# Waiting for a low part at the third matmul of a chunk in a three-layer kernel

## What is computed

```python
def _moe_ref(x, w_gate, w1, w2):
    ...                          # greedy assignment of 384 tokens to each expert
    for e in range(E):
        mask = assigned == e
        h = np.maximum(x[mask] @ w1[e], 0.0)
        out[mask] = h @ w2[e]

def _moe2_ref(x, w_gate, w_val, w_out):
    g = x @ w_gate
    silu = g * (1.0 / (1.0 + np.exp(-g)))
    val = x @ w_val
    return (silu * val @ w_out).astype(np.float32)
```

## Time and profile before

| | |
|---|---|
| median of 3 runs | 854.0 us (853.72 to 854.21) |
| the profiled execution | 853.57 us, span 851.7 us |
| TensorE busy | 821.5 us, 96% of the span, 6116 matmuls |
| TensorE weight loads busy | 784.0 us, 92% |
| VectorE, ScalarE, GpSimd busy | 508.2 us (60%), 299.1 us (35%), 235.7 us (28%) |
| of the 85.50 us from 273.00 to 358.50 (one expert's turn) | TensorE 85.35, weight loads 83.67, VectorE 48.11, ScalarE 28.05, GpSimd 22.03; granted clock 1.00 |
| largest shares of the chain that ended last | `ps_up` L1775 48%, `ps_acc` L1775 28% |

### The profile page before, as it was taken

One profiled execution on the slowest core, in us unless ns is written; L12 is line 12 of the kernel. 1 busy time (PEld: TensorE's weight loads), 2 busy tenths in 40 slices (PEclk: granted clock), 3 DMA queues, 4 the chain that ended last, 5 costly groups with the idle time before them and its releaser, 6 DMA issues.

```text
span 851.7 us, 16768 instructions
## 1 busy us (share of the span) xinstructions
PE 821.5 (96%) x6116; PEld 784.0 (92%) x6116; DVE 508.2 (60%) x1095; ACT 299.1 (35%) x607; POOL 235.7 (28%) x263
## 2 busy tenths in 40 slices
PE   9999993899999999999999999999999999999995
PEld 5888882699999999999999999999999999999995
DVE  9999987746554655465546554655466546642332
ACT  2566652432343234322432333233323332333221
POOL 3222210388613041304130413041305040504001
PEclk9999996899999999999999999999999999999998
DMA  8898852402300230023002300230023002300000
GB/s 292 280 328 286 288 174 77 147 1 75 103 27 1 74 102 20 8 74 102 18 9 74 102 18 9 74 102 18 9 74 102 18 9 74 102 19 11 0 1 32
DMA packets 25858, 70.98 MB, mean 83 GB/s; under 512 B 3808, under 2 KB 10464, under 8 KB 25824
## 3 DMA queue, kind: packets, MB, share of 16 engines
q1 hardware_dynamic: 19296, 56.39, 20.2%
q0 software_dynamic: 3072, 9.44, 3.4%
q10 hardware_dynamic: 3456, 4.72, 1.5%
HBM read 61.10 MB, written 9.44 MB: 83 GB/s over the span
## 4 chain that ended last, share of the span: by engine, by line
PE 80%; DVE 2%; ACT 1%; issue 1%; POOLq 0%; POOL 0%; DVEq 0%; ACTq 0%
PE ps_up L1775 48%; PE ps_acc L1775 28%; PE ps_up L1868 1%; PE ps_turn_again L1002 1%; PE ps_turn_again L1023 1%; PE ps_turn L1781 1%; DVE z_low L1720 1%; ACT z_high L1654 0%; PE ps_turn_again L840 0%; DVE quick_at_row L922 0%; DVE quick_at_row L809 0%; PE ps_up L1781 0%; POOLq L1908 0%; DVE x_low L1761 0%; DVE quick_base L822 0%
## 5 line engine op out<-in xcount | busy, mean ns | idle before, releaser
L1775 PE MATMUL ps_up<-z_high,gated_high 128*128 128x384 f32 x576 | 197.8, 343 | 1.5 <-DVE z_low L1720 1.5
L1775 PE MATMUL ps_up<-z_high,gated_low 128*128 128x384 f32 x576 | 195.0, 339 | 0.0
L1775 PE MATMUL ps_up<-z_low,gated_high 128*128 128x384 f32 x576 | 192.9, 335 | 0.0
L1560 POOL TENSOR_TENSOR w_low<-w_raw,w_high 128x384 fp32r<-128x384 f32 x120 | 118.5, 1013 | 251.3 <-ACT w_high L1641 251.0
L1775 PEld LDWEIGHTS ps_up<-z_high,gated_high 128*128 128x128 f32 x576 | 108.2, 188 | 3.0 <-issue 2.1
L1725 DVE TENSOR_TENSOR act_out<-ps_up,act_out 128x384 f32<-128x384 f32 x96 | 53.4, 556 | 92.4 <-ACT act_out L1657 90.7
L1775 PEld LDWEIGHTS ps_up<-z_high,gated_low 128*128 128x128 f32 x576 | 108.3, 188 | 0.0
L1775 PEld LDWEIGHTS ps_up<-z_low,gated_high 128*128 128x128 f32 x576 | 108.1, 188 | 0.0
L1660 ACT CAST u_high<-ps_up 128x384 fp32r<-128x384 f32 x96 | 46.0, 479 | 169.6 <-DVE ps_up L1729 169.6
L1657 ACT ACTIVATE act_out<-ps_up 128x384 f32<-128x384 f32 x96 | 47.1, 490 | 144.8 <-PE ps_up L1775 144.8
L1775 PE MATMUL ps_acc<-gated_high,u_high 128*128 128x384 f32 x288 | 97.3, 338 | 0.3 <-DVE u_low L1732 0.3
(11 more groups left out here) (220 smaller groups left out, 1420.3 us busy)
## 6 DMA issues: line engine op xcount, KB each, us to landing
w_raw<-in_experts SPq DMA_DIRECT2D x64, 384.0 KB, 3.0
qka_in<-in_qka SPq DMA_DIRECT2D x22, 770.5 KB, 5.7
gated_raw<-in_gated SPq DMA_DIRECT2D x12, 576.0 KB, 6.2
v_in<-in_v SPq DMA_DIRECT2D x24, 192.0 KB, 5.2
x_rows<-y_rows ACTq DMA_DIRECT2D x24, 192.0 KB, 4.4
qka_in<-in_qka SPq DMA_DIRECT2D x2, 512.0 KB, 4.7
qka_in<-in_qka SPq DMA_DIRECT2D x2, 258.5 KB, 3.4
out<-o_tok,to_rows POOLq DMA_INDIRECT x24
```

Source lines behind the costliest of these rows:

```text
L1560: part = pool.tensor_tensor(w.low[:, m % RING, cols], w.raw[:, m % RING, cols], w.high[:, m % RING, cols].bitcast(F32), ALU.subtract)
L1775: mm = pe.matmul(acc, lhs[a], rhs[b], start=(first and i == 0), stop=(last and i == 2))
```

## The change

Before, each place that reads a split operand for the first time waits for both of its parts ahead of the first of the three matmuls. After, it waits for the high part there, and `product` waits for the low part ahead of the third matmul, which is the only one to read it. This holds for x at the three slices of up(0), for h at each down chunk, for z at the three slices of the first gate chunk, and for u at each projection chunk. In the projection u stands on the left, where its low part was read by the second matmul; there the second and the third matmul change places (`low_of == "lhs"`). The values and what is summed stay as they are.

```diff
@@ -1769,9 +1769,12 @@
             expert(E - 1, last=True)
 
         def tensor(pe):
-            def product(acc, lhs, rhs, first, last):
-
-                for i, (a, b) in enumerate(((0, 0), (1, 0), (0, 1))):
+            def product(acc, lhs, rhs, first, last, low_of, low_ready=None, count=None):
+
+                parts = ((0, 0), (1, 0), (0, 1)) if low_of == "rhs" else ((0, 0), (0, 1), (1, 0))
+                for i, (a, b) in enumerate(parts):
+                    if i == 2 and low_ready is not None:
+                        pe.wait_ge(low_ready, count)
                     mm = pe.matmul(acc, lhs[a], rhs[b], start=(first and i == 0), stop=(last and i == 2))
                 return mm
 
@@ -1785,19 +1788,19 @@
                 for k in range(K1):
                     if m == 0:
                         pe.wait_ge(x_high_ready, K1 * e + k + 1)
-                        pe.wait_ge(x_low_ready, K1 * e + k + 1)
                     cols = slice(k * P, (k + 1) * P)
                     mm = product(ps_up[m % 2][0][:, 0:CAP], (w.high[:, m % RING, cols], w.low[:, m % RING, cols]),
-                                 (x_high[:, k, :], x_low[:, k, :]), k == 0, k == K1 - 1)
+                                 (x_high[:, k, :], x_low[:, k, :]), k == 0, k == K1 - 1, "rhs",
+                                 x_low_ready if m == 0 else None, K1 * e + k + 1)
                 mm.then_inc(h_ready, 1)
 
             def down(e, m):
                 pe.wait_ge(h_high_ready, FC * e + m + 1)
-                pe.wait_ge(h_low_ready, FC * e + m + 1)
                 for k in range(K1):
                     cols = slice(DM + k * P, DM + (k + 1) * P)
                     mm = product(ps_acc[k][:, 0:CAP], (w.high[:, m % RING, cols], w.low[:, m % RING, cols]),
-                                 (h_high[:, m % 2, :], h_low[:, m % 2, :]), m == 0, m == FC - 1)
+                                 (h_high[:, m % 2, :], h_low[:, m % 2, :]), m == 0, m == FC - 1, "rhs",
+                                 h_low_ready if k == 0 else None, FC * e + m + 1)
                     if m == FC - 1:
                         mm.then_inc(z_ready, 1)
                 if m < RING:
@@ -1807,22 +1810,22 @@
                 pe.wait_ge(w.gated_low_ready, j + 1)
                 for g, ready in ((0, g_ready), (1, v_ready)):
                     for k in range(K1):
-                        if j == 0 and g == 0:
+                        starting = j == 0 and g == 0
+                        if starting:
                             pe.wait_ge(z_high_ready, K1 * e + k + 1)
-                            pe.wait_ge(z_low_ready, K1 * e + k + 1)
                         cols = slice(g * DM + k * P, g * DM + (k + 1) * P)
                         mm = product(ps_up[j % 2][g][:, 0:CAP], (w.gated_high[:, j, cols], w.gated_low[:, j, cols]),
-                                     (z_high[:, k, :], z_low[:, k, :]), k == 0, k == K1 - 1)
+                                     (z_high[:, k, :], z_low[:, k, :]), k == 0, k == K1 - 1, "rhs",
+                                     z_low_ready if starting else None, K1 * e + k + 1)
                     mm.then_inc(ready, 1)
 
             def project(e, j):
                 pe.wait_ge(u_high_ready, GC * e + j + 1)
-                pe.wait_ge(u_low_ready, GC * e + j + 1)
                 for t in range(T3):
                     cols = slice(t * P, (t + 1) * P)
                     mm = product(ps_acc[t][:, 0:DM], (u_high[:, j % 2, cols], u_low[:, j % 2, cols]),
                                  (w.gated_high[:, j, 2 * DM:3 * DM], w.gated_low[:, j, 2 * DM:3 * DM]),
-                                 j == 0, j == GC - 1)
+                                 j == 0, j == GC - 1, "lhs", u_low_ready if t == 0 else None, GC * e + j + 1)
                     if j == GC - 1:
                         mm.then_inc(o_ready, 1)
```

## The result

The median of 5 runs went from 853.72 us (853.37 to 854.21) to 849.45 us (849.17 to 849.57): a ratio of 0.9949, with a 95% interval of 0.9938 to 0.996. The profiled execution took 849.57 us with a span of 847.7, against 853.57 and 851.7: 4.0 us less in both. The forecast was 850.7, 0.996. Direction and places were right, the size was not: 3.3 us were expected of the profiled execution, 4.0 came, and the median of before was 0.3 lower than the 854.0 that the forecast started from.

The account below looks back on a forecast made before the run. TensorE, busy for 96% of the span, was taken as the bound. 2.17 + 3 x 0.38 = 3.3 us off the profiled 853.57 gives 850.3; with the median 0.4 above, 850.7 us (0.996), 8-in-10 range 849.4 to 852.4.

Parts of the forecast that it names:

- The mechanism: TensorE's waits for low parts move two matmuls later, 208 in all; only places where it stands idle gain.
- the ten places: Seven gate starts, last expert's gate, first product, last projection: TensorE idles there today; 3.3 us to be gained.
- The swapped order: Projection's second and third matmul exchanged, 864 matmuls: taken as 0, with 1.0 us kept either way.
- The waits that are met: The other places of the 208, where the wait is met in time: cost taken at zero.
- the mark that should have shown that something else was gained: Time from one expert's first gate matmul to the next expert's should be 0.31 us shorter.
- The seven gates: Gate's start in seven experts with a routing step: 0.79 to 0.48 us, 7 x 0.31 = 2.17 us.
- The three small places: Last expert's gate, first product of all, last projection: 0.38 us gained at each.
- the mark that it named: Nine matmuls of a projection should still take 1.57 us; 1.56 or 1.59 would mean the swap has its own price.
- Paid again: Rival: third waits met at the last moment pay a restart of 0.09 at 28 places; 853.2 us, chance 0.09.
- Given back: Rival: something not started from TensorE sets a later point, so the gain is lost; 854.0 us, chance 0.08.
- Slower: Rival: a wait inside a chunk stops loads made ahead, 208 places pay 0.09 each; 869.4 us, chance 0.04.
- A worse pace of the projection: Rival: swapped projections' pace worse by more than a us, the gain still there; 852.3 us, chance 0.03.

Follow-up runs that it names:

- without the swap: The whole change except the projection's part, which keeps its old order and old waits, against the kernel before: 850.6 us, 0.9967.
- the runs with the two writes: Extra VectorE write ahead of z's first subtraction: 96 columns in both kernels (changed 849.5 us, before 856.23), 320 in the changed kernel (850.67).
- the kernel with the low part's wait alone: Kernel before, with only the low part's wait kept at each chunk's head and the high part's separate wait dropped: 853.7 us, 0.9997.
- the old order and the late wait: Changed kernel, projection in its old order with the wait for u's low part at its second matmul: 850.27 us, 0.9962 against before.
- the 720 waits: Changed kernel plus 720 long-met waits ahead of third matmuls in up, gate and value slices: 849.61 us, 0.9949 against before.
- 0.6 lost for the gate: Changed kernel with second and third matmul also exchanged in gate and value chunks, except each expert's first gate chunk: 849.97 us, 0.9953 against before.
- the kernel before with the short write: Kernel before plus a 96-column VectorE write ahead of each expert's first z subtraction: 856.23 us in one profiled execution.
- the idle matmuls: Changed kernel plus three idle matmuls between the first rows' transposes, and low parts read one matmul later in last gate and projection: 849.35 us, 0.9947.

## What of the prediction held, and which steps failed

The mechanism held: the ten places and nothing else stopped waiting, and they gave what was forecast for them. The forecast failed in its sum, which came out at 3.3 us of the profiled execution where 4.0 went. Two terms that it had put at nothing made the difference. The swapped order of the projection, taken as 0, is worth 0.45 us, in the chunks behind the projections. The waits that are met, taken as 0, are worth 0.17 us at the eight first down chunks. Another 0.05 us, in the gate and value chunks, came without the swap too, and its cause is open.

**The mechanism.** The steps for the gate held one by one: 0.79 to 0.48, the second matmul of the gate where it was computed, the third load on time, nothing paid again. From one expert's first gate matmul to the next's it was 358.53 - 272.93 = 85.60 us and is 85.20. Changed kernel, timeline, the third expert's first gate matmul (the second expert's is at 271.96, above):

```profile
357.16 0.42 PE L1778 MATMUL ps_up<-z_high,gated_high 128*128 128x384 f32 x1
```

0.40 less, where 0.31 was said: the mark that should have shown that something else was gained as well, in each expert, and did.

**The seven gates** gave 2.08 for 2.17: 0.31 at the second matmul as forecast, 0.013 given back later in the chunk.

**The three small places** were taken at 0.38 within 0.35 to 0.45 and gave 0.45, 0.42 and 0.40. The first is 0.39 if it is counted by x's low part, as said above. The term failed where it let the load go 0.11 after its producer, as behind the separate instruction in the earlier trace rows. With the wait on the load itself it goes 0.04 to 0.06 after it (160.21 against 160.17 at the start, 782.10 against 782.05 at the last gate). The working had named this and chosen the other end. It is 0.07 to 0.13 us too little. That the ten places add up as forecast is in part luck, since the seven gates were taken 0.09 too high. The stretch that a load may be late, 0.07, taken from one row, held in every run: 0.11 late cost 0.04, 0.18 cost 0.10, 0.25 cost 0.18, 0.35 cost 0.28. The last gates of the runs with the two writes fit too: 0.15 late cost 0.08, 0.38 cost 0.31. For 6 places in 4 kernels the loss is the lateness less 0.07, within 0.01.

Behind a late load the matmul after its own starts 0.28 after the load in four kernels (837.32 to 837.60 above). Less one spacing of 0.174 that is 0.106, and 0.174 less 0.106 is the 0.07 to spare.

The Trainium skill ("TensorE: Matmul & The Clock Gate", section on LDWEIGHTS) puts a load at its columns over 1.2 GHz, which gives an estimate of 107 ns for 128 columns. The traces agree with it by their 0.106.

**"A wait that is met costs nothing."** This step failed for separate waits that are met just ahead of their turn, and held for those met earlier, for those behind a routing step and for those inside a chunk. The earlier trace rows was read at one matmul, whose start is on time; the 0.013 to 0.027 us come at the matmuls behind it, up to the seventh. They make 0.17 us in the eight first down chunks (and 0.03 at the last expert's last one); the kernel with the low part's wait alone gave the same 0.17 with no wait moved. A place is judged over the chunk, not by the next start.

**The swapped order** was taken as 0, with 1.0 either way (the 288 that the prediction calls chunks are groups of three matmuls, three in each of 96 chunks). It gives 0.45 us by the changed kernel against the one without the swap (0.34 in the gate and value chunks, 0.15 in the first up chunks, less 0.04 in the projections). It was within the 1.0 that was kept for it, and it was the largest part of the miss. The reason given for 0 was that projection and down chunks pair their loads differently and both show 1.57; it put the whole effect on the projections' own spacing. So the mark that it named, whether nine of them take 1.57 us or 1.56, could point to an effect but not measure it. The chain of the changed kernel, to be read against the earlier trace rows (start us, us, engine, tile, line, count):

```profile
312.59 1.57 PE ps_acc L1778 x9
...
317.31 1.56 PE ps_acc L1778 x9
```

Of the stretches of nine in this chain 26 take 1.56 and 33 take 1.57; in the chain of before none takes 1.56. Yet over all projections, start to start, nothing was gained: some chunks are up to 0.005 shorter and others as much longer, and the step into them is longer on the whole. What was gained is at what follows a projection. The medians point the same way (849.45 with all of it, 850.27 with the old order and the late wait, 850.6 without the projection's part), though their intervals overlap; the stages of the traces are the stronger evidence.

**The starting point.** 854.0 was the median of 3 runs; 5 runs gave 853.72. With it the forecast of 0.996 would have been 850.4.

**The rivals.** Paid again: no, a late load costs its lateness and no restart, and the chunks' third loads are on time. Given back: no, the time moved by as much as the sum of the places, and no new wait is in the list. Slower: no, by the 720 waits, whose stages took the same time within 0.02 us. A worse pace of the projection: no, in the other direction.

## What to carry to other kernels

Where a product is made of several matmuls on parts of one operand, put each wait at the first matmul that reads its part and put that matmul last: at the places where the part is there the wait costs nothing that could be seen here, and it gives the whole of the gap where it is late, as long as the late load comes no more than 0.07 us after its turn (for matmuls of 384 columns, as here). To find such a gap, compare the start-to-start distance over the place with an equal place where nothing is late. When an edit reorders matmuls, measure the stretch behind them too, since a change of pace may show in the next stage rather than in the one that was edited.

## What the runs showed of the hardware

**A late weight load has 0.07 us to spare**, for these matmuls of 384 columns, spaced 0.174. Beyond that the lateness is paid one for one (0.11 late cost 0.04, 0.38 cost 0.31).

**A separate wait instruction on TensorE can cost though it is met**: 0.013 to 0.027 us at the nine down chunks where it is met 0.11 us ahead of its turn, spread over the next matmuls, and 0.01 us in all at the other 150 places in down and projection chunks. It lets a waiting load go 0.11 after its producer's end where a wait on the load lets it go at 0.04 to 0.06.

**The order of two matmuls changes the spacing of later ones**, 0.45 us gained over 3744 matmuls for the projection, 0.6 lost for the gate. Why is open: no view shows what differs, and the two orders load the same weights equally often.

**TensorE's clock fell to half at the first product in two of fourteen profiles**: in the kernel with the low part's wait alone and in the kernel before with the short write. Profile of the first in stretches (window, its length, then busy us and instructions of TensorE, weight loads, VectorE, ScalarE, GpSimd; the granted clock; DMA share, GB/s):

```profile
157.20:160.90 3.70, 1.84 (x12) 1.13 (x11) 3.22 (x11) 2.08 (x6) 0.10 (x1) 1.00 0.37 100
161.00:164.30 3.30, 3.30 (x12) 3.30 (x11) 0.51 (x2) 1.16 (x2) 0.00 (x0) 0.50 0.94 301
```

The changed kernel, the same two stretches and the one ahead of them:

```profile
155.00:157.20 2.20, 2.20 (x8) 0.84 (x7) 2.10 (x6) 0.00 (x0) 1.90 (x2) 0.72 0.47 123
157.20:160.90 3.70, 2.92 (x18) 1.98 (x17) 3.30 (x12) 1.85 (x6) 0.20 (x1) 1.00 0.35 100
161.00:164.30 3.30, 3.30 (x20) 3.30 (x20) 1.56 (x6) 1.78 (x3) 0.00 (x0) 1.00 0.90 304
```

At a granted clock of 0.50, which is 1.2 of 2.4 GHz, 12 matmuls start in 3.3 us where 20 do at 1.00: 1.6 us lost over the stages. Ahead of the fall TensorE was busy for 1.84 of the 3.70 us in which it waits for the gathered rows (2.92 in the changed kernel).

Every profile has a longer stretch of half clock ahead of this place, through the routing, where TensorE is busy for under half of the time (8.33 of the 21.50 us from 132.50 to 154.00 in the changed kernel, at a granted clock of 0.50). In nine of the fourteen it ends at 155.5 to 157.2, in the changed kernel at 156.2, which is the 0.72 of its first row. In five it ends earlier, at 154.1 to 155.0, and two of these five are the ones that fell again at the first product. Where the clock came back early and stayed, as in the second profile of the changed kernel, no loss shows: its first product starts at 160.16, against 160.21.

The fall may be why runs of the kernel before spread (852.8 to 855.3 over the 25), where the changed kernel's ten stay within 849.1 to 849.7; that is not shown, since only profiles show where the clock fell. Whether the earlier start of the first product makes the fall rarer, and whether the idle matmuls prevent it, no run shows either, as neither profile of the changed kernel nor that of the version with them has the fall.
